# Two of a score tile's four matmuls contract over 64 rows in the two row halves of the TensorE array, and tanh is written in place

## The reference

```python
scores = (1 / sqrt(64)) * q @ k.T                    # q, k, v: 4 batches, 8 heads, 576 positions, 64 dims
scores = scores + bias[head, i, j]                   # a small MLP of |i - j| and i
attn = softmax(scores)                               # over keys
x = (attn @ v)                                       # laid out as 2304 tokens x 512
h = x @ moe_w_in;  y = (h - tanh(h)) @ moe_w_out     # 512 -> 2048 -> 512
out = (silu(y @ w_gate) * (y @ w_val)) @ moe2_w_out  # 512 -> 1536 -> 512
```

## Time and profile before

| | before |
|---|---|
| median of 3 runs | 1286.54 us (1286.43 to 1287.05) |
| the profiled execution's own time | 1287.1 us |
| its span in the trace | 1285.3 us |
| mean granted TensorE clock | 0.98 |

### The profile page before, as it was taken

One profiled execution on the slowest core, in us unless ns is written; L12 is line 12 of the kernel. 1 busy time (PEld: TensorE's weight loads), 2 busy tenths in 40 slices (PEclk: granted clock), 3 DMA queues, 4 the chain that ended last, 5 costly groups with the idle time before them and its releaser, 6 DMA issues.

```text
span 1285.3 us, 25567 instructions
## 1 busy us (share of the span) xinstructions
PE 1202.0 (94%) x8400; PEld 1133.1 (88%) x8400; DVE 639.4 (50%) x1592; ACT 593.3 (46%) x1285; POOL 556.2 (43%) x656
## 2 busy tenths in 40 slices
PE   4656689999999999999999999999999999999997
PEld 2236689999999999999999999999999999999997
DVE  8976766666666666666666653521211212112111
ACT  6876645565655655656556555521212222122211
POOL 0007757677677676776776743311111111111111
PEclk9897889999999999999999999999999999999999
DMA  6875534444344444443444434400000000000000
GB/s 179 242 233 178 159 94 126 123 130 122 111 141 123 128 123 124 127 126 108 141 124 129 125 113 166 142 25 1 25 25 27 25 23 27 1 25 1 25 1 25
DMA packets 69375, 125.02 MB, mean 97 GB/s; under 512 B 8768, under 2 KB 32320, under 8 KB 69312
## 3 DMA queue, kind: packets, MB, share of 16 engines
q1 hardware_dynamic: 69312, 124.16, 32.7%
HBM read 104.07 MB, written 20.05 MB: 97 GB/s over the span
## 4 chain that ended last, share of the span: by engine, by line
PE 48%; issue 33%; POOL 8%; DVE 7%; ACT 3%; DMA 1%; POOLq 0%; SPq 0%; DVEq 0%; ACTq 0%
PE ps_h L995 14%; PE ps_y L1012 13%; PE ps_s L950 7%; PE ps_pt L963 6%; POOL fr L513 5%; PE ps_pt L973 5%; DVE feat L733 2%; PE ps_y L973 1%; DVE wbuf L725 1%; POOL prob L479 1%; POOL fr L484 1%; DVE prob L759 1%; ACT wbuf L564 1%; DVE wbuf L774 1%; DVE wbuf L720 1%
## 5 line engine op out<-in xcount | busy, mean ns | idle before, releaser
L513 POOL TENSOR_TENSOR fr<-x_stage,fr 128x384 fp32r<-128x384 f32 x72 | 73.0, 1014 | 382.4 <-ACT fr L679 382.4
L1012 PE MATMUL ps_y<-fr,wbuf 128*128 128x288 f32 x1536 | 225.4, 295 | 1.1 <-POOL fr L484 0.4
L995 PE MATMUL ps_h<-fr,wbuf 128*128 128x288 f32 x1440 | 220.1, 296 | 0.7 <-DVE fr L801 0.7
L1012 PEld LDWEIGHTS ps_y<-fr,wbuf 128*128 128x128 f32 x1536 | 210.3, 188 | 2.9 <-POOL fr L484 2.7
L479 POOL TENSOR_SCALAR prob<-prob,rowinv 96x576 f32<-96x576 f32 x192 | 145.1, 762 | 142.1 <-DVE rowinv L769 141.4
L995 PEld LDWEIGHTS ps_h<-fr,wbuf 128*128 128x128 f32 x1440 | 201.1, 189 | 1.6 <-issue 0.9
L774 DVE TENSOR_TENSOR wbuf<-ps_pt,wbuf 128x480 fp32r<-128x480 f32 x176 | 115.8, 658 | 166.2 <-ACT wbuf L564 165.5
L564 ACT ACTIVATE wbuf<-ps_pt 128x480 fp32r<-128x480 f32 x176 | 100.7, 572 | 199.8 <-PE ps_pt L963 199.4
L1094 PE MATMUL ps_y<-wbuf,fr 128*128 128x512 f32 x648 | 162.5, 395 | 1.3 <-POOL fr L513 1.3
L556 ACT ACTIVATE prob<-prob,negmax 96x576 f32<-96x576 f32 x192 | 147.8, 770 | 5.9 <-DVE negmax L759 5.4
L484 POOL TENSOR_TENSOR fr<-g_b,fr 128x288 fp32r<-128x288 f32 x128 | 112.4, 878 | 81.3 <-ACT fr L574 81.3
(11 more groups left out here) (107 smaller groups left out, 1829.5 us busy)
## 6 DMA issues: line engine op xcount, KB each, us to landing
biasb<-bias_scratch SPq DMA_DIRECT2D x192, 216.0 KB, 3.9
k_raw<-k_t SPq DMA_DIRECT2D x63, 288.0 KB, 2.8
v_raw<-v_p SPq DMA_DIRECT2D x64, 160.0 KB, 3.4
q_raw<-q_t SPq DMA_DIRECT2D x64, 144.0 KB, 2.5
biasb<-w_chunks SPq DMA_DIRECT2D x32, 256.0 KB, 3.7
prob<-w_chunks SPq DMA_DIRECT2D x8, 768.0 KB, 4.3
bias_scratch<-x_stage SPq DMA_DIRECT2D x36, 144.0 KB, 2.6
bias_scratch<-y_stage SPq DMA_DIRECT2D x36, 144.0 KB, 2.6
```

The source lines that it names most:

```text
L513: eng.tensor_tensor(a_lo[c % 2], a_b, a_hi[c % 2].bitcast(F32), ALU.subtract).then_inc(p_alo, 1)
L995: mm = eng.matmul(hidden_bank(u, c)[:, 0:T1], w[:, cols], x[:, d, :], start=d == 0 and i == 0, stop=d == KC - 1 and i == 2)
L1012: mm = eng.matmul(ps_y[:, d, 0:T1], w[:, cols], g[c % 2], start=c == 0 and i == 0, stop=c == C1 - 1 and i == 2)
```

## The change

Of the four matmuls of a score tile the two with `k_hi` stay as they were. The two with `k_lo` no longer contract over all 128 rows: each uses 64 rows, those with q's high part alone. The left half of the keys (a = 0) uses rows 0 to 63 of `q` and of `k_lo`, and the right half (a = 1) uses rows 64 to 127 of `k_lo` and of a new tile `q_up`, whose rows 64 to 127 hold q's high part as well. So the product q low times k low is no longer computed. `q_up` is written by a second ACT instruction of 64 partitions behind `q_high`, with a semaphore `a_qup` of its own, for which PE waits at t = 0, and SP before it loads the next q. Its room in SBUF is that of `tanh_b`, which goes: tanh now writes to `g_b[:, i, :]`, and `gated` subtracts in place there. With that the wait for `split_g` two chunks back moves from `gated` (DVE) to `tanh` (ACT), and the wait of `tanh` for the `gated` before it goes.

```diff
+        q_even_up = fr[:, at + 2 * S + T1:at + 2 * S + 2 * T1]
...
-        tanh_b = sb("tanh_b", [P, T1])
+        q_up = sb("q_up", [P, T1], F32R)
...
-            return (q_even, *k_even) if moe is None and par == 0 else (qq, k_hi, k_lo)
+            return (q_even, q_even_up, *k_even) if moe is None and par == 0 else (qq, q_up, k_hi, k_lo)
...
             def load_q(n):
                 wait(eng, v_q, n)
+                wait(eng, a_qup, n)
...
-                eng.activation(operands(par, moe)[0], q_raw[:, :], ACT.Copy, scale=float(D) ** -0.5).then_inc(a_q, 1)
+                q, q_upper, _, _ = operands(par, moe)
+                eng.activation(q, q_raw[:, :], ACT.Copy, scale=float(D) ** -0.5).then_inc(a_q, 1)
+                eng.activation(q_upper[D:P, :], q_raw[D:P, :], ACT.Copy, scale=float(D) ** -0.5).then_inc(a_qup, 1)
...
-            def tanh(m, bank):
+            def tanh(m, i, bank):
                 eng.wait_ge(e_h, m + 1)
-                eng.wait_ge(v_g, m + CR)
-                eng.activation(tanh_b[:, :], bank[:, 0:T1], ACT.Tanh).then_inc(a_tanh, 1)
+                eng.wait_ge(p_glo, m + (CR - 1))
+                eng.activation(g_b[:, i, :], bank[:, 0:T1], ACT.Tanh).then_inc(a_tanh, 1)
...
             def gated(m, i, bank):
                 eng.wait_ge(a_tanh, m + 1)
-                eng.wait_ge(p_glo, m + (CR - 1))
-                eng.tensor_tensor(g_b[:, i, :], bank[:, 0:T1], tanh_b[:, :], ALU.subtract).then_inc(v_g, 1)
+                eng.tensor_tensor(g_b[:, i, :], bank[:, 0:T1], g_b[:, i, :], ALU.subtract).then_inc(v_g, 1)
...
             def scores(n, par, t, moe):
-                q, *ks = operands(par, moe)
+                q, q_upper, hi, lo = operands(par, moe)
                 bank = score_bank(par, t, moe)
                 if t == 0:
                     eng.wait_ge(p_klo, n + 1)
                     eng.wait_ge(v_q, n + 1)
+                    eng.wait_ge(a_qup, n + 1)
 
                 wait(eng, v_score, n * NQ + (t if moe is not None else t - 1))
-                for i, k in enumerate(ks):
-                    for a in range(2):
-                        mm = eng.matmul(bank[0:QT, a, 0:T1], q[:, t * QT:(t + 1) * QT], k[:, a * T1:(a + 1) * T1],
-                                        start=i == 0, stop=i == 1)
+                rows = slice(t * QT, (t + 1) * QT)
+                for a in range(2):
+                    eng.matmul(bank[0:QT, a, 0:T1], q[:, rows], hi[:, a * T1:(a + 1) * T1], start=True, stop=False)
+                for a, part in enumerate((q[0:D, rows], q_upper[D:P, rows])):
+                    mm = eng.matmul(bank[0:QT, a, 0:T1], part, lo[a * D:(a + 1) * D, a * T1:(a + 1) * T1],
+                                    start=False, stop=True)
                 mm.then_inc(e_score, 1)
```

More of the change, by code:

```diff
@@ L166, in attention_layers_kernel @@
         e_pt, a_pt, v_pt, e_o, a_o, v_x = (sem(x) for x in ("e_pt", "a_pt", "v_pt", "e_o", "a_o", "v_x"))
-        a_q, v_q, p_khi, p_klo, p_vhi, p_vlo = (sem(x) for x in ("a_q", "v_q", "p_khi", "p_klo", "p_vhi", "p_vlo"))
+        a_q, a_qup, v_q, p_khi, p_klo, p_vhi, p_vlo = (sem(x) for x in ("a_q", "a_qup", "v_q", "p_khi", "p_klo", "p_vhi", "p_vlo"))
         v_xhi, v_xlo = sem("v_xhi"), sem("v_xlo")
@@ L457, in split_k @@
                 eng.wait_ge(d_k, n * 16 + 16)
-                _, hi, lo = operands(par, moe)
+                _, _, hi, lo = operands(par, moe)
                 wait(eng, e_score, preparing(n, moe))
@@ L619, in slot @@
                 if moe is not None:
-                    tanh(m, hidden_bank(moe[0], 0))
+                    tanh(m, 0, hidden_bank(moe[0], 0))
                 if pv:
@@ L631, in slot @@
                 if late:
-                    tanh(m + 1, hidden_bank(moe[0], 1))
+                    tanh(m + 1, 1, hidden_bank(moe[0], 1))
                 if prep:
```

## The result

The changed kernel takes 1331.97 us (median of 4 runs, 1327.72 to 1332.03), against 1286.49 us (1286.22 to 1287.05): the ratio over all runs, which is not quite that of the medians, is 1.0347, with a 95% interval of 1.0334 to 1.0359. It is slower by 45.5 us. The forecast was 1269 and is wrong. The time lies between the two prices of rival 1, 1323 and 1381, and inside the wide range up to 1335, whose upper part was there for that rival.

The account below looks back on a forecast made before the run. PE was taken to bound the stretch where attention and first layer run together. 16.8 us for 165 tiles plus 1.0 us for the attention-only stage, 17.8 off 1287.1, gave 1269 us; case range 1264 to 1280, whole range 1264 to 1335.

Parts of the forecast that it names:

- rival 1: The array runs empty at each switch of array shape: 1323 us, or 1381 with weight loads exposed; chance 0.41.
- What bounds the kernel: With attention and first layer together, PE is busy 584.6 of 591.0 us, so a nanosecond off PE comes off the end.
- The pair: Two 64-row score matmuls stream side by side with 30 ns lag: 102 ns saved a tile, 16.8 us over 165 tiles.
- The switch: Two changes a tile between whole array and halves: bounded by 0 and 677 ns together, taken as nothing.
- the rival's sign: If the array empties, a tile's first half starts some 290 ns after the matmul before; slot 11.2 us or more.
- The attention-only stage: Before the layer starts, five score groups in the chain at a low clock save about 1.0 us, between 0 and 1.2.
- ScalarE's copy: The new ACT instruction, 0.41 us a slot, ends in two idle stretches of 0.79 us and costs nothing.
- tanh in place: Writing tanh to g_b costs nothing: its new wait, for split_g one slot earlier, is over long before.
- k's remainder: POOL ends it at 414.59, scores load weights at 414.83; PE gains 0.10 of that 0.24 us, so it holds.
- rival 3: POOL's remainder of k becomes the bound: at most 0.07 us a slot lost, 3.9 us, 1273 us; within the forecast's 0.47.
- Rival 2: No change: halves take turns or switches eat the pair's gain; 1286.5 us, within 2.6 us; chance 0.12.

Follow-up runs that it names:

- 96-row run: The changed kernel with both remainder matmuls of a tile over 96 rows and no row halves: 1291.98 us, ratio 1.0042.
- same-half run: The changed kernel with both 64-row matmuls of a tile in the same half of the array, rows 0 to 63: 1356.06 us, ratio 1.0541.
- full-rows run: The changed kernel with all four score matmuls over 128 rows again, q's upper copy and tanh in place kept: 1291.52 us, ratio 1.0041.

## Why the prediction was wrong

- **What bounds the kernel:** right. PE's row is full in the layer stage, and each nanosecond put on it came out at the end.
- **The pair:** right, and mis-sized against me. The lag is 3 ns (median over 108 tiles), not 30, so a tile saves nearly the whole turn of 132 ns, not 102.
- **The switch: the step that failed.** The term that I put at nothing ("For the forecast I take nothing") measured 0.37 us a tile, 0.185 for each of its two switches. Of the bound I gave, 677 ns for the two, 370 came true. The ground I gave, that weight loads of other strips start a few ns apart and that 96 to 128 rows is free, concerned one shape both times, as the 96-row run shows.
- **Rival 1** foresaw the loss and very nearly its size: 224 ns a tile and 37.0 us, where 240 ns a tile and 39.6 us in the layer stage were measured. That its first price came so close is partly luck. It took the whole 163 ns in flight for each switch and no weight load. The same-half run shows 90 ns for the late start and 80 or 110 ns for a weight load. The first half starts 0.22 us behind the matmul before it, not the 0.29 of the rival's sign. The rule that a change of tiling mode drains TensorE (the Trainium skill, TensorEngine Tiling (Array Packing), Key Properties) agrees with the trace in that each change costs time, 0.185 us on average. The rival should have had more than 0.41, since nothing in the trace spoke against it.
- **The attention-only stage:** forecast as 1.0 us saved, measured 5.9 us lost, of which 5.2 by halves alone. I left out the switches there too, and what the halves do to the clock.
- **ScalarE's copy:** "cost nothing" failed. In the full-rows run it costs 3.6 us in six second slots, of 5.1 us over before. There are six such slots and not seven, since the first unit has no results to copy. I read the idle time of one ordinary slot, and at a unit's end I looked at the last slot but not the first, which holds `y_out`. In the changed kernel these waits are shorter, 6 of 0.4 us, since PE itself comes later.
- **tanh in place:** right, 0.9996. **k's remainder, rival 3:** no wait of that kind shows. **Rival 2:** out; the halves don't take turns.
- **Sum as measured:** 165 x 0.24 = 39.6 us for the tiles and 5.9 us for the attention-only stage make 45.5. That this is the measured difference to the tenth is luck: 0.24 is rounded, and the copy's waits in the layer stage, 6 x 0.4 us, come on top; shorter waits on POOL at unit ends (4.6 us in all, before 5.4) take back some of them, and the rest I did not take apart.

## What to carry to other kernels

Two 64-row matmuls in the two row halves take one turn for two, but moving into and out of that shape costs 0.37 us here, nearly three turns of 288 columns. From this I estimate that it pays only if three or more pairs stand together (3 x 0.132 = 0.40 us saved). One pair a tile lost 0.24 us and two pairs lost 0.11; three were not run, nor were the pairs of a slot's three tiles put side by side. A shape that the trace never shows under load has an unknown price, and with a bound of 0 to 677 ns against a gain of 102 the unknown decides. Cover for an added instruction is read in the fullest slot of a loop, not in an ordinary one.

## What the runs showed of the hardware

- A switch between the whole array and row halves cost 0.18 to 0.19 us beyond the turns at the full clock, as an average over both directions, in four arrangements. It has two parts: the first matmul behind it starts 0.09 us late, its weight load no longer under the matmul before, and the one after that waits for an exposed weight load, 0.11 us with 128 columns and 0.08 us with 96. Weight load and matmul start together there, so the traces don't say which of the two holds up the other.
- Row halves in two banks of PSUM start 3 ns apart (median). Two matmuls in the same half, right behind a switch, start 0.21 us apart. 96 rows behave as the whole array.
- In the attention-only stage the granted clock averaged 0.80 before and 0.69 in the changed kernel. PE's busy time there rose from 50.5 to 62.6 us, in part because a matmul takes longer at the lower clock; a lower clock came with more busy time and not with less.
